# Four of the six additions of a tile's convolution done by accumulating DMAs, in two of 32 tiles

## The reference

```python
w = softmax(weight_gen, axis=-1)                 # 7 taps for each of 8 heads of 24 columns
x_pad = 6 rows of zeros ahead of each sequence
out[b, s, h, :] = sum over k of w[b, s, h, k] * x_pad[b, s + k, h, :]    # causal convolution
hid = out.reshape(16384, 192) @ w_in
g   = np.maximum(0.01 * hid, hid)
return g @ w_out                                 # 16384 x 192
```

## Time and profile before

| | us | share of the span |
|---|---|---|
| median of 3 runs | 1035.06 | |
| profiled execution, first to last instruction (span) | 1033.8 | |
| TensorE busy (PE) | 1024.1 | 99% |
| VectorE busy (DVE) | 945.2 | 91% |
| ScalarE busy (ACT) | 631.1 | 61% |
| GpSimd busy (POOL) | 545.6 | 53% |

### The profile page before, as it was taken

How to read it: one execution, slowest core, us unless ns; L and a number is a source line. 1 busy time by engine, 2 the same in 40 slices (tenths; PEclk the granted TensorE clock), 3 DMA queues, 4 the chain that set the end, 5 groups by cost and what they waited for, 6 DMA issues and landing times.

```text
span 1033.8 us, 28952 instructions
## 1 busy us (share of the span) xinstructions
PE 1024.1 (99%) x12755; PEld 614.6 (59%) x12755; DVE 945.2 (91%) x1227; ACT 631.1 (61%) x1332; POOL 545.6 (53%) x369
## 2 busy tenths in 40 slices
PE   8999999999999999999999999999999999999998
PEld 4666566555655655655665565565565565556566
DVE  7999999999999999999999999999999999998611
ACT  6766566566556656565665565665566565566554
POOL 0004556545655665665565665565566556556543
PEclk9999999999999999999999999999999999999999
DMA  9101213112131310213211131210313102111100
GB/s 264 65 16 32 87 30 97 35 32 81 20 97 35 95 34 19 83 34 97 35 33 66 35 98 34 72 56 6 97 34 97 35 22 76 35 35 35 35 17 17
DMA packets 67445, 57.48 MB, mean 56 GB/s; under 512 B 56252, under 2 KB 60604, under 8 KB 65336
## 3 DMA queue, kind: packets, MB, share of 16 engines
q1 hardware_dynamic: 67196, 55.35, 19.1%
q10 hardware_dynamic: 124, 0.29, 0.1%
HBM read 29.34 MB, written 12.58 MB: 41 GB/s over the span
## 4 chain that ended last, share of the span: by engine, by line
PE 90%; DVE 6%; SPq 1%; DMA 1%; ACT 1%; issue 0%; POOL 0%; DVEq 0%; ACTq 0%; POOLq 0%
PE h_ps L969 43%; PE out_ps L1079 22%; PE t_ps L1079 22%; DVE conv L612 1%; DVE prod L605 1%; PE out_ps L1033 1%; DVE gl L654 1%; PE h_ps L951 1%; DMA rawD<-in_moe_w_in_dram 1%; PE out_ps L1043 1%; SPq L329 1%; DVE xs L644 0%; DVE xs L642 0%; SPq L332 0%; DVE wo L634 0%
## 5 line engine op out<-in xcount | busy, mean ns | idle before, releaser
L298 POOL TENSOR_TENSOR gl<-g,gh 128x512 f16<-128x512 f32 x360 | 543.6, 1537 | 479.7 <-ACT g L426 479.7
L424 ACT ACTIVATE gh<-h_ps 128x512 f16<-128x512 f32 x512 | 317.4, 620 | 373.8 <-PE h_ps L969 360.9
L1079 PE MATMUL t_ps<-wo,gh 64*128 64x384 f16 (+1 forms) x1984 | 386.6, 317 | 0.9 <-ACT gh L424 0.9
L1079 PE MATMUL out_ps<-wo,gh 64*128 64x384 f16 (+1 forms) x1984 | 386.6, 317 | 0.0
L969 PE MATMUL h_ps<-xT,whA 64*128 64x512 f16 x1920 | 364.3, 376 | 0.0
L426 ACT ACTIVATE g<-h_ps 128x512 f32<-128x512 f32 x512 | 321.8, 628 | 0.0
L612 DVE TENSOR_TENSOR conv<-conv,prod 128x768 f32<-128x768 f32 x186 | 277.8, 1493 | 1.1
L605 DVE TENSOR_TENSOR prod<-xbuf,taps 128x768 f32<-128x768 f32 x186 | 273.6, 1483 | 0.0
L1079 PE MATMUL t_ps<-wo,gl 64*128 64x192 f16 x1920 | 233.2, 243 | 1.4 <-DVE gl L654 1.4
L1079 PE MATMUL out_ps<-wo,gl 64*128 64x192 f16 x1920 | 233.2, 243 | 0.0
L1079 PEld LDWEIGHTS t_ps<-wo,gh 64*128 64x128 f16 x1984 | 181.3, 94 | 57.7 <-ACT gh L424 1.4
(11 more groups left out here) (99 smaller groups left out, 681.3 us busy)
## 6 DMA issues: line engine op xcount, KB each, us to landing
xbuf<-in_x_dram SPq DMA_DIRECT2D x15, 1344.0 KB, 6.0
out_dram<-stage SPq DMA_DIRECT2D x31, 384.0 KB, 2.4
taps<-in_weight_gen_dram SPq DMA_DIRECT2D x16, 224.0 KB, 5.9
xT_again<-xT SPq DMA_DIRECT2D x29, 64.0 KB, 2.1
rawO<-in_moe_w_out_dram SPq DMA_DIRECT2D x4, 384.0 KB, 10.0
rawA<-in_moe_w_in_dram SPq DMA_DIRECT2D x2, 512.0 KB, 8.4
xbuf<-in_x_dram SPq DMA_DIRECT2D x2, 384.0 KB, 6.6
rawD<-in_moe_w_in_dram SPq DMA_DIRECT2D x1, 512.0 KB, 7.3
```

The source lines that it names most:

```text
L298: nc.gpsimd.tensor_tensor(gl[:, f % RING, :], g[:, f % RING, :], gh[:, f % RING, :], ALU.subtract).then_inc(s_gl_p, 1)
L424: nc.scalar.activation(gh[:, f % RING, :], h_ps[f % GROUP][:], ACT.Prelu, scale=SHRINK, alpha=SLOPE).then_inc(s_gh, 1)
L1079: ins = nc.tensor.matmul(dst, a[rows, f % RING, j * P:(j + 1) * P], moved, start=i == 0 and k < 2 and a is gh and f == 0 and part != 1, st ...
```

## The change

For tiles 1 and 2 `CONV` is replaced by a list `QUEUED` with seven products in a row, two additions and the same five last steps. GpSimd issues four DMAs that add one buffer to another in SBUF (384 KB each): product 1 is added to `conv`, product 3 to product 2's buffer, product 5 to product 4's, and then product 2's buffer (2 + 3) to `conv`. VectorE adds product 4's buffer (4 + 5) and product 6. `prod` has six buffers instead of three. The other tiles keep `CONV`. The waits on `s_conv` are counted with the new lengths, and the groups of gl and weight pieces stand at other places between the steps.

```diff
+QUEUED = ([("mul", k) for k in range(7)] + [("sum", 3), ("sum", 5)]
+          + [(what, 0) for what in ("top", "mask", "unscale", "scale", "out_scale")])
+QUEUED_TILES = (1, 2)
...
-        prod = sb("prod", [P, PRODS, SUB * D])
+        prod = sb("prod", [P, 6, SUB * D])
...
+            def add_products(t):
+
+                i, acc = QUEUED_TILES.index(t), conv[:].rearrange("p j d -> p (j d)")
+                pool.wait_ge(s_conv, conv_done(t, ("mul", 1)))
+                nc.gpsimd.dma_start(acc, prod[:, 0, :], accum_op=ALU.add).then_inc(s_add_first, DMA)
+                pool.wait_ge(s_conv, conv_done(t, ("mul", 3)))
+                nc.gpsimd.dma_start(prod[:, 1, :], prod[:, 2, :], accum_op=ALU.add).then_inc(s_add_next, DMA)
+                pool.wait_ge(s_conv, conv_done(t, ("mul", 5)))
+                nc.gpsimd.dma_start(prod[:, 3, :], prod[:, 4, :], accum_op=ALU.add).then_inc(s_add_last, DMA)
+                pool.wait_ge(s_add_first, DMA * (2 * i + 1))
+                pool.wait_ge(s_add_next, DMA * (i + 1))
+                nc.gpsimd.dma_start(acc, prod[:, 1, :], accum_op=ALU.add).then_inc(s_add_first, DMA)
+
+            for t in QUEUED_TILES:
+                add_products(t)
...
-                    sp.wait_ge(s_conv, m * N_CONV + CONV.index(("mul", K - 1)) + 1)
+                    sp.wait_ge(s_conv, conv_done(m + 1, ("mul", K - 1)))
                     load_chunk(c + 2, c % 2)
...
                 if what == "mul":
-                    if k > PRODS:
-
-                        dve.wait_ge(s_conv, N_CONV * (t - 1) + CONV.index(("add", k - PRODS)) + 1)
+                    if k > PRODS and t not in QUEUED_TILES:
+
+                        dve.wait_ge(s_conv, conv_done(t, ("add", k - PRODS)))
...
+                elif what == "sum":
+
+                    i = QUEUED_TILES.index(t)
+                    if k == 3:
+                        dve.wait_ge(s_add_first, DMA * 2 * (i + 1))
+                        dve.wait_ge(s_add_last, DMA * (i + 1))
+                    dve.wait_ge(s_conv, conv_before(t) + n)
+                    ins = nc.vector.tensor_tensor(acc, acc, prod[:, k, :], ALU.add)
...
-                conv1(3, 4)
+                early_conv(1, ("mul", 3))
                 lo_pieces(4, 5)
-                conv1(4, 5)
+                early_conv(1, ("mul", 4))
                 group(0)
                 lo_pieces(5, 7)
-                conv1(5, 9)
+                early_conv(1, ("mul", 5), ("mul", 6))
                 lo_pieces(7, 8)
-                conv1(9, 11)
                 group(1)
                 lo_pieces(8, 10)
-                conv1(11, N_CONV)
+                early_conv(1, ("sum", 3), ("out_scale", 0))
                 lo_pieces(10, 11)
                 lo_of_x(1)
                 group(2)
...
-                for n in range(4):
-                    convolve(2, n)
+                early_conv(2, ("mul", 0), ("mul", 3))
                 group(NG)
-                for n in range(4, 9):
-                    convolve(2, n)
+                early_conv(2, ("mul", 4), ("mul", 6))
                 group(NG + 1)
-                for n in range(9, N_CONV):
-                    convolve(2, n)
+                early_conv(2, ("sum", 3), ("out_scale", 0))
                 group(NG + 2)
                 lo_of_x(2)
```

More of the change, by code:

```diff
@@ L36, with conv_of, conv_before, conv_done @@
 N_CONV = len(CONV)
-SCALED = CONV.index(("scale", 0)) + 1
+QUEUED = ([("mul", k) for k in range(7)] + [("sum", 3), ("sum", 5)]
+          + [(what, 0) for what in ("top", "mask", "unscale", "scale", "out_scale")])
+QUEUED_TILES = (1, 2)
 N_SOFTMAX = 6
+def conv_of(t):
+    return QUEUED if t in QUEUED_TILES else CONV
+def conv_before(t):
+    return sum(len(conv_of(u)) for u in range(1, t))
+def conv_done(t, op):
+    return conv_before(t) + conv_of(t).index(op) + 1
 CONV_TO = (4, 8, CONV.index(("top", 0)))
@@ L153, in dynconv_mlp @@
         s_conv = sem("s_conv")
+        s_add_first = sem("s_add_first")
+        s_add_next = sem("s_add_next")
+        s_add_last = sem("s_add_last")
         s_x_hi = sem("s_x_hi")
@@ L404, in hi_of_x @@
                 else:
[L405 removed]
+                    act.wait_ge(s_conv, conv_done(t, ("scale", 0)))
                     if t > BY_PE:
@@ L435, in copy_out @@
                 else:
-                    act.wait_ge(s_conv, N_CONV * m)
+                    act.wait_ge(s_conv, conv_before(m + 1))
                 if wide(m):
@@ L593, in convolve @@
                 odd, buf = t % 2, t // 2 % 2
-                what, k = CONV[n]
+                what, k = conv_of(t)[n]
+                acc = conv[:].rearrange("p j d -> p (j d)")
                 if n == 0:
@@ L603, in convolve @@
                     w = taps[:, buf, :].rearrange("p (r k) -> p r k", k=K)[:, SUB * odd * H:SUB * (odd + 1) * H, k:k + 1]
-                    dst = conv[:].rearrange("p j d -> p (j d)") if k == 0 else prod[:, k % PRODS, :]
+                    dst = acc if k == 0 else prod[:, k - 1 if t in QUEUED_TILES else k % PRODS, :]
                     ins = nc.vector.tensor_tensor(dst.rearrange("p (r g) -> p r g", g=G), rows,
                                                   w.to_broadcast([P, SUB * H, G]), ALU.mult)
+                elif what == "sum":
[5 more added lines that the diff above has]
+                    ins = nc.vector.tensor_tensor(acc, acc, prod[:, k, :], ALU.add)
                 elif what == "add":
                     done = max(CONV.index(("mul", k)), CONV.index(("add", k - 1) if k > 1 else ("mul", 0)))
-                    dve.wait_ge(s_conv, N_CONV * (t - 1) + done + 1)
-                    acc = conv[:].rearrange("p j d -> p (j d)")
+                    dve.wait_ge(s_conv, conv_before(t) + done + 1)
                     ins = nc.vector.tensor_tensor(acc, acc, prod[:, k % PRODS, :], ALU.add)
                 else:
-                    dve.wait_ge(s_conv, N_CONV * (t - 1) + n)
+                    dve.wait_ge(s_conv, conv_before(t) + n)
                     if what == "top":
@@ L783, in lo_pieces, with early_conv @@
                     split_lo(piece)
-            def conv1(first, last):
-                for n in range(first, last):
-                    convolve(1, n)
+            def early_conv(t, first, last=None):
+                ops = conv_of(t)
+                for n in range(ops.index(first), ops.index(last or first) + 1):
+                    convolve(t, n)
             def group(n):
@@ L797, in first_tile @@
                 dve.wait_ge(s_chunk[0], DMA)
-                conv1(0, 1)
+                early_conv(1, ("mul", 0))
                 lo_pieces(2, 4)
-                conv1(1, 2)
+                early_conv(1, ("mul", 1))
                 w_top(1)
-                conv1(2, 3)
+                early_conv(1, ("mul", 2))
                 w_scales(1)
```

## The result

The changed kernel takes 1041.16 us (median of 18 runs, 1039.87 to 1044.14), the kernel before 1035.03 (18 runs, 1034.44 to 1039.55). The ratio is 1.0053, 95% interval 1.0043 to 1.0062: slower by half a per cent, where I had forecast 0.9 us less. The profiled execution of the changed kernel has a span of 1038.9 us, 5.1 more than before.

The account below looks back on a forecast made before the run. TensorE was taken as the bound, so only its waits of 0.27 + 0.39 + 0.2 = 0.86 us could be won: 1035.06 - 0.86 = 1034.2 us. The range was 1033.0 to 1044.0.

Parts of the forecast that it names:

- What bounds the kernel: TensorE, busy 1024.1 of 1033.8 us: time is won only where it stands idle, 0.86 us in all.
- the gap of 0.27, the 0.39 in the gl block and the 0.2 for x: TensorE's waits near 49 to 53 us and for tile 2's transposed x, all winnable: 0.86 us.
- VectorE's relief: In tiles 1 and 2, 3.5 us leave VectorE per tile; it reaches tile 1's first sum at 40.9, not 44.35.
- Issue of 1.26 us: Time one accumulating DMA's issue keeps GpSimd: 1.26 us, bounds 0.33 and 2.09.
- Landing of 3.7 alone: Time for an accumulating DMA to land with nothing beside it: 3.7 us, bounds 2.1 to 10.0.
- the margin of 1.7 us: Tile 2's last accumulation was to land at 72.9, 1.7 us before the sums at 74.59.
- I add half of this, 2 us: Tile 1's fourth DMA: 2 us added for SP's load of the next chunk, which fills the DMA engines some 4 us.
- A wait paid one to one: At each tile's first sum, a late landing is paid in full, once per tile, and never recovered.
- I cost the gaps at 193 and 234 as unchanged: TensorE's later gaps, 0.89 and 1.35 us, stay, since VectorE's lead can't pass 125 us.
- The slower rival: Late landings bound each tile's first sum, the fourth DMA waiting for the second: +15.8 us, 1050.9; chance 0.22.
- L = 7.2: Issue-to-landing time, nothing beside it, from which late landings in both tiles decide: a loss of 5.1 us.
- The lock between an issue and VectorE: Each GpSimd issue slows one VectorE instruction from 0.95 to 1.91 us: +0.3 per tile, 1035.7; chance 0.05.

Follow-up runs that it names:

- the later load: Changed kernel, but SP's load of chunk 2 waits for tile 1's third and fourth accumulating DMAs: 1034.13 us, ratio 0.9998 to the kernel before.
- tile 1 alone: Changed kernel with only tile 1 queued, tile 2 in its old order, and the load of chunk 2 waiting for tile 1's accumulations: 1034.10 us, ratio 0.9989.
- the filled wait: Changed kernel with 18 matmuls of zeros before TensorE waits for the third piece of w_out: 1039.93 us, ratio 1.0051 to the kernel before.
- the swapped order: Changed kernel with GpSimd issuing the accumulation into conv (the fourth) ahead of that of products 4 and 5: 1041.01 us, ratio 1.0057.
- tile 2 alone: Changed kernel with only tile 2 queued, tile 1 keeping its six additions on VectorE: 1039.81 us, ratio 1.0053 to the kernel before.
- the sums ahead: Kernel with only tile 2 queued, VectorE's four sums in tile 5 moved ahead of softmax steps and gl: 1039.26 us, ratio 1.0028.

## Why the prediction was wrong

- **What bounds the kernel**: right. TensorE won nothing where it doesn't wait, and the gap of 0.27, the 0.39 in the gl block and the 0.2 for x are what a version in time gets back: 0.66 us between the medians with the later load, and the ratio 0.9989 with tile 1 alone, its interval just clear of 1.
- **VectorE's relief**: right. First sum at 40.9 by my steps; VectorE was free at 39.9 in an execution that began 1.1 earlier.
- **Issue of 1.26 us**: 0.86 to 1.21. **Landing of 3.7 alone**: 4.1 by itself; the fourth took 5.5 in tile 1 with the later load, behind the third, and 4.6 to 6.5 in tile 2. Both were near enough with the later load, where all lands in time; in tile 2 the margin of 1.7 us did not hold in the four kernels where one DMA engine was late.
- **The step that failed: "I add half of this, 2 us"**, the term for the load beside tile 1's fourth DMA. It is 11.9 us to landing instead of 5.7; against the 5.5 measured without the load, the term is 6.4 us, of which one late DMA engine has 1.3. I had noted that product 6 releases the load 4.4 us earlier, and that it meets the fourth DMA; I took the load for 4 us of work to be shared, and only with the fourth. The trace shows that it slows the third first (6.3 us of packets instead of 2.2), that the fourth's packets come behind the third's, and that it then shares with the rest of the load. The later load, which takes the collision away (and lets the fourth end before the next instruction fetch), removes the loss.
- **A wait paid one to one**: right for the wait, wrong for its price. The sums came 2.8 us later by the clock and TensorE's block 2.8 us later. To this came 2.4 us, because the granted clock was 0.5 for the block behind 4.67 us of idleness. I hadn't costed the clock at all, and a row for it was at hand: the half clock at 28 us in the kernel before. Filling the wait brought the clock back; that this brings all of the 2.4 us in time is not shown.
- **"I cost the gaps at 193 and 234 as unchanged"**: right for a lead, and for the changed kernel. As a rule it was wrong in the other direction: a lead of VectorE ends at 125 us, but the kernel before stands next to a point from which one more collision with GpSimd grows into a gap of 4.3. I had the rows (0.1 us of idle at 125, the doubled instructions) and read them for one sign only.
- **The slower rival** had the right place and engine (the landings at the first sum). It wanted L = 7.2 in both tiles; it was one tile, with 11.9. That 1041.2 lies inside my range of 1033.0 to 1044.0 is therefore luck: the range reached there through this rival's slow landings in both tiles, with the load at 2 us and the clock at nothing.
- **The lock between an issue and VectorE**: it doesn't happen. VectorE's instructions beside the issues keep 0.95.

Still open: why the changed kernel, whose tile 2 was in time in the profiled execution, varies from 1039.9 to 1044.1, and the kernel before from 1034.3 to 1041.0. Three sources are in the traces: the start (the matmul of w_spread began between 24.9 and 27.9 us, in four kernels with half clock behind it, and tile 1 alone with the later load, profiled at 1036.97, had nearly all its delay there), the landings of tile 2, which differ by 1.9 us between kernels (below), and the step at GpSimd's subtractions. Only one execution of each kernel is profiled, so which of them makes a given time is not shown.

## What to carry to other kernels

Where a step is handed to a DMA, look at what its producers release besides: here the same product released the accumulation and a load of four times its bytes, and one wait on the load's side was worth some 6 us. A DMA in the path of a result should have the DMA engines to itself, and the DMA ahead of it in its queue counts as part of it. Before moving work that a busy engine needs back by a given time, test with one dummy instruction what a small lateness costs; in this kernel 0.95 us on VectorE costs about 4, because it tips which engine comes first at a collision. Compare such kernels at the place where they part, and not by the sum of their busy times, which hid the half clock here.

## What was not expected of the hardware

- Half clock: after 4.67 us without a matmul TensorE's granted clock was 0.5 until about 57 us, and a block of 2.81 us took 5.24. The length of the last gap alone doesn't tell: after single gaps of 0.9 to 1.6 us near 193 and 235 us it stayed at 1.0, after waits of 1.33 and 0.47 us at 26 to 27 us (the kernel before) it fell to 0.5, and in the swapped order it stayed at 1.0 after 1.71, 0.47 and 0.85.
- Who comes first: two instructions that start within 0.1 us of each other, one on VectorE and one on GpSimd, decide by their order which of them is held up (0.94 or 1.91 us for the same product).
- An accumulation within SBUF costs twice a store's time per packet (0.27 to 0.12 us), and alternates packet by packet with a load whose packets are longer.
- In four kernels (tile 2 alone, with and without the sums ahead, the filled wait, the swapped order) one of the 16 DMA engines finished tile 2's last accumulation 1.2 to 1.4 us behind the other fifteen (for example at 74.9, the others by 73.5), and each time a fetch of 16 KB of instructions, 0.9 to 1.0 us long, was in progress before that engine was done. So it was with tile 1's last accumulation in the changed kernel (46.7, the others by 45.4). In tile 2 of the changed kernel and of the one with the later load the fetch came after the last packet, and no engine was late: landing 4.6 instead of 5.8 to 6.5 us. The Trainium skill (DMA: Bandwidth & Descriptors, Why a DMA increments its semaphore by 16 and not by 1) says that each engine posts its own share and only the full count means landed; the trace agrees, the slowest engine decides. That the fetch is the cause is read off these traces, and no run tested it.
